# A fused attention and two-layer MoE kernel: the first MoE's first product by seven block products instead of eight, with the second product two pairs behind

## The reference

```python
def sm_attn(qq, kk, vv):
    s = scale * np.matmul(qq, kk.transpose(0, 1, 3, 2))
    s = s - np.max(s, axis=-1, keepdims=True)
    a = np.exp(s)
    a = a / (np.sum(a, axis=-1, keepdims=True) + 1e-09)
    return np.matmul(a, vv)
p_packed = sm_attn(p, k, v)               # batch 8, heads 8, 32 packed queries, keys 576, head_dim 64
x = sm_attn(q, p_packed, p_packed)        # then laid out as 4608 tokens x 512

h = x @ w_in                              # first MoE: 512 -> 2048
x1 = (h - np.tanh(h)) @ w_out             # 2048 -> 512
h = x1 @ w_in2                            # second MoE
r = np.maximum(h, 0.0)
y = (s * (r * r) + b) @ w_out2
```

## Time and profile before

| | us |
|---|---|
| median of 3 runs (lowest to highest) | 1444.14 (1443.78 to 1445.14) |
| the profiled execution's own time | 1444.17 |
| its span, first to last instruction | 1442.3 |
| PE, DVE, ACT busy in the span | 1431.0, 826.2, 548.2 |

### The profile page before, as it was taken

How to read it: one execution, slowest core, us unless ns; L and a number is a source line. 1 busy time by engine, 2 the same in 40 slices (tenths; PEclk the granted TensorE clock), 3 DMA queues, 4 the chain that set the end, 5 groups by cost and what they waited for, 6 DMA issues and landing times.

```text
span 1442.3 us, 22038 instructions
## 1 busy us (share of the span) xinstructions
PE 1431.0 (99%) x8584; PEld 1189.7 (82%) x8584; DVE 826.2 (57%) x1442; ACT 548.2 (38%) x996; POOL 78.0 (5%) x71
## 2 busy tenths in 40 slices
PE   8999999999999999999999999999999999999998
PEld 6788887878788888888898888888888888888887
DVE  7565555555555555764667455844557455754553
ACT  3444343443443343443344223722235223632243
POOL 2242010100101000000000000000000000000000
PEclk9999999999999999999999999999999999999999
DMA  9898777687877754668697644865466644756145
GB/s 347 283 309 298 237 239 267 226 289 234 276 251 255 241 179 148 225 231 286 232 360 271 240 166 180 280 227 220 180 235 234 254 170 174 279 214 245 59 131 190
DMA packets 128807, 337.51 MB, mean 234 GB/s; under 512 B 22976, under 2 KB 46656, under 8 KB 124096
## 3 DMA queue, kind: packets, MB, share of 16 engines
q1 hardware_dynamic: 128560, 336.04, 66.5%
q10 hardware_dynamic: 144, 0.07, 0.0%
HBM read 282.07 MB, written 54.00 MB: 233 GB/s over the span
## 4 chain that ended last, share of the span: by engine, by line
PE 97%; DMA 1%; DVE 1%; SPq 0%; ACT 0%; issue 0%; DVEq 0%; ACTq 0%
PE banks L304 31%; PE banks L305 31%; PE banks L306 30%; PE banks L675 2%; DMA qT<-q_T 1%; PE banks L617 1%; PE banks L639 1%; PE banks L694 1%; PE banks L625 0%; SPq L362 0%; ACT g_high L933 0%; DVE g L1308 0%; DVE w_in_first L1249 0%; PE banks L603 0%; PE banks L648 0%
## 5 line engine op out<-in xcount | busy, mean ns | idle before, releaser
L304 PE MATMUL banks<-g_high,w_out_ring 128*128 128x512 f32 x1152 | 456.8, 397 | 0.4 <-DVE g_low L1232 0.4
L305 PE MATMUL banks<-g_low,w_out_ring 128*128 128x512 f32 x1152 | 449.3, 390 | 0.0
L306 PE MATMUL banks<-g_high,w_out_ring 128*128 128x512 f32 x1152 | 448.7, 390 | 0.0
L304 PEld LDWEIGHTS banks<-g_high,w_out_ring 128*128 128x128 f32 x1152 | 216.3, 188 | 73.1 <-issue 15.8
L306 PEld LDWEIGHTS banks<-g_high,w_out_ring 128*128 128x128 f32 x1152 | 216.4, 188 | 46.1
L305 PEld LDWEIGHTS banks<-g_low,w_out_ring 128*128 128x128 f32 x1152 | 216.5, 188 | 40.1
L1308 DVE TENSOR_TENSOR g<-banks,tanh 128x288 f32<-128x288 f32 x256 | 115.9, 453 | 232.2 <-ACT tanh L973 231.9
L1033 ACT ACTIVATE g<-g,small 128x512 f32<-128x512 f32 x144 | 117.4, 815 | 295.0 <-DVE g L1398 294.3
L973 ACT ACTIVATE tanh<-banks 128x288 f32<-128x288 f32 x256 | 105.4, 412 | 281.2 <-PE banks L306 279.1
L304 PE MATMUL banks<-x_operands_wide,w_in_first 128*128 128x512 f32 x448 | 174.3, 389 | 0.0
L305 PE MATMUL banks<-x_operands_wide,w_in_first 128*128 128x512 f32 x448 | 174.3, 389 | 0.0
(11 more groups left out here) (146 smaller groups left out, 1458.2 us busy)
## 6 DMA issues: line engine op xcount, KB each, us to landing
w_out_ring<-w_out_parts_scratch SPq DMA_DIRECT2D x272, 512.0 KB, 4.1
w_in_first<-w_in_operands_scratch SPq DMA_DIRECT2D x28, 1792.0 KB, 7.3
w_in_ring<-w_in SPq DMA_DIRECT2D x30, 1024.0 KB, 6.4
kT<-k_T SPq DMA_DIRECT2D x16, 576.0 KB, 7.0
qT<-q_T SPq DMA_DIRECT2D x16, 576.0 KB, 5.9
x1T_scratch<-out_store SPq DMA_DIRECT2D x9, 1024.0 KB, 7.5
v_rows<-v_rows SPq DMA_DIRECT2D x8, 1024.0 KB, 6.5
w_out_parts_scratch<-w_out_ring SPq DMA_DIRECT2D x16, 512.0 KB, 4.7
```

Source lines behind the costliest of these rows:

```text
L304: nc.tensor.matmul(out, high, rhigh, start=first, stop=False)
L305: nc.tensor.matmul(out, high, rlow, start=False, stop=False)
L306: return nc.tensor.matmul(out, low, rhigh, start=False, stop=last)
```

## The change

The loop over steps becomes a loop over 64 pairs of feature chunks (8 in a batch; p is the pair, q its place in the batch). The first four pairs are done as before, with 16 steps called `plain`. In each of the other 60 the 2x2 blocks (two inner blocks, two chunks by two inner blocks, two token halves) go by seven products instead of eight, 21 matmuls of 288 columns instead of 24. Of these:

- the operands are seven blocks each, made by DVE: for M in `m_round` and `m_sums` (in two pairs `m_round` once and `m_sums` twice), for the softmax weights in `at_mix` and `at_lows` (once in a batch);
- the products are summed partly in PSUM: ACT copies the first product from bank 4 to bank 6 (`move_p1`), a product is added on top, ACT copies that to bank 7 (`move_u2`), and the next are added on both. The product in bank 5 is copied to SBUF (`copy_p5`) and DVE adds it in (`add_pair`);
- the second product runs two pairs behind, `second_d` giving its four output blocks one at a time between the seven products; g is kept in a ring of four pairs, and every pair's leftover tokens are stored on their own;
- banks 4 to 7 are all taken by the pair, so the side work (`side`, `side_late`) borrows banks 4 and 5 between the last product of one pair and the first of the next, and `side_free` makes PE wait until they are read.

```diff
+LAG = 2
+            def side_late(p):
+                b, q = divmod(p, PF)
+                if q == 1 and b + 1 < B:
+                    pe.wait_ge(turn2_done, 2 * b + 2)
+                    if b + 2 < B:
+                        pe.wait_ge(s1_out, s1_copied(b + 2) + 2)
+                    scores2(2 * b + 3)
...
+                if q == 7 and b + 2 < B:
+                    if b + 3 < B:
+                        pe.wait_ge(s1_out, s1_copied(b + 3) + 1)
+                    packed_t(2 * b + 4)
+                    packed_t(2 * b + 5)
+            def pair(p):
...
+                side_free(p - 1, C11)
+                prod(C11, 0, 0, True, True).then_inc(p1_done, 1)
+                second_d(a, 0)
+                pe.wait_ge(p1_moved, k + 1)
+                pe.wait_ge(mb_ready, 4 * n + 3 + p % 2)
+                prod(U2B, 4, 5, False, True).then_inc(u2_done, 1)
+                prod(C11, 1, 1, False, True).then_inc(c11_done, 1)
+                second_d(a, 1)
+                pe.wait_ge(u2_moved, k + 1)
+                wait(pe, p5_copied, k)
+                side_free(p - 1, P5)
+                prod(P5, 3, 4, True, True).then_inc(p5_done, 1)
+                prod(U3B, 5, 6, False, True).then_inc(p7_done, 1)
+                prod(U2B, 6, 3, False, True).then_inc(p3_done, 1)
+                second_d(a, 2)
+                second_d(a, 3)
+                pe.wait_ge(add_done, 2 * k + 1)
+                prod(U3B, 2, 2, False, True).then_inc(p4_done, 1)
+                side(p)
+                second_d(a + 1, 0)
+                second_d(a + 1, 1)
+                second_d(a + 1, 2)
+                side_late(p)
+                second_d(a + 1, 3)
...
+            def move_p1(p):
...
+                nc.scalar.copy(banks[:, U2B, 0:U1], banks[:, C11, 0:U1]).then_inc(p1_moved, 1)
...
+                move_p1(p)
+                high_g1(2 * (p - 1))
+                move_u2(p)
+                tanh_pair(p, 0)
+                high_g1(2 * (p - 1) + 1)
+                copy_p5(p)
+                if q % 2 == 1 and (p - 1) // 2 + 1 < ROUNDS and p > PLAIN:
+                    m_sums((p - 1) // 2 + 1, 0)
+                    m_sums((p - 1) // 2 + 1, 1)
+                if b + 1 < B and q == 3:
+                    exp2(nxt)
+                for i in range(1, 4):
+                    tanh_pair(p, i)
...
+                low_g1(2 * (p - 1))
+                minus_pair(p, 0)
+                low_g1(2 * (p - 1) + 1)
...
+                if 1 <= b < B - 1 and q == 2:
+                    max2_(nxt)
+                    sub2(nxt)
+                if 1 <= b < B - 2 and q == 4:
+                    max1(nxt + 2)
+                    max1(nxt + 3)
+                add_pair(p)
+                for i in range(1, 4):
+                    minus_pair(p, i)
```

1027 lines of the change are left out of this document (607 added, 420 removed).

## The result

The changed kernel takes 1528.78 us (median of 4, 1523.22 to 1532.7) against 1444.57 (1443.78 to 1445.14) for the kernel before in the same comparison: ratio 1.058, 95% interval 1.0544 to 1.0617. It is 84 us slower, where 32 were forecast. The profiled execution has a span of 1529.7 us.

The account below looks back on a forecast made before the run. PE's work, busy 1431.0 of 1442.3 us, was taken to bound the kernel. 1442.3 - 23.9 removed + 53 of waits + 3 at the start = 1474.4 of span, 1476 with the 1.9 around it; range 1452 to 1490.

Parts of the forecast that it names:

- The matmuls removed: On PE, 60 pairs lose three matmuls of 288 columns, 0.1325 us each: 23.9 us saved, 3.2 in a batch.
- DVE's work: Per batch, DVE gets 21 us more than 43.5, about 65 where PE needs 76.8; fits on average.
- Rival 3: Bank copy or PSUM traffic is dear: `move_p1` at 0.6 us bites in 60 pairs, 18 more, 1494; chance 0.06.
- Places A to C: Three spots in a batch where PE waits behind softmax work; with 0.3 at q = 6, 7.6 us a full batch.
- B: Pair q = 7, batches 0 to 4: PE waits 2.1 us before the packed rows' transposes, 0.15 more behind them.
- place A: Pairs q = 3 and 4, batches 1 to 5: softmax work on DVE delays the addition; PE waits 2.7 us.
- Rival 4: The clock falls in pauses, each under 3 us; a batch at 1.2 GHz would add some 77; chance 0.02.
- The ninth block: End of the first MoE's second product: no wait of its own; second product and transfers costed at nothing.
- The start: Before pair 4, M's low parts share VectorE with the softmax: 3 us more waiting, between 0 and 8.
- The pairs: Waits in the 60 changed pairs: 8.9 us in batch 0, 7.6 each in batches 1 to 4; 53 in all.
- Range: Whole kernel: 1452 to 1490 us, reaching over most of rival 2 and some way towards rival 3.
- Rival 2: Half the waits: ACT and DVE overlap more, or a place is misplaced; 27 to 38 us, 1447 to 1461; chance 0.15.

Follow-up runs that it names:

- adds_first: Changed kernel with softmax maxima and subtraction on VectorE put behind the additions and subtractions in pairs 2 and 4 of each full batch; 1508.88 us, ratio 1.0448.
- norms_first: Changed kernel with `norm1` ahead of `m_sums` in pair 7 and `at_lows` moved to the end of pair 6 on VectorE; 1508.46 us, ratio 1.0444.
- hold_sooner: Changed kernel plus useless TensorE products inside the pauses of pairs 4 and 7, the latter ahead of the scores copy wait; 1519.88 us, ratio 1.0519.
- all_orders: Changed kernel with `adds_first`, `norms_first`, earlier left-column loads, later x-operand work in the ninth block, and `turn2` ahead of `m_sums` in pair 1; 1480.54 us.
- best: `all_orders` plus a GpSimd wait before the fifth w_out split, earlier low parts of the start's last weight pair, and useless products in batch 0's pauses; 1477.16 us.
- after_again: The changed kernel itself measured once more, nothing edited; 1526.57 us, ratio 1.0569 against the kernel before.
- left_only: Changed kernel with only the loads of g's left columns issued two second products earlier; 1524.37 us, ratio 1.0565.

## Why the prediction was wrong

The direction and the mechanism were right, the size was not: 1528.8 is outside 1452 to 1490. Step by step, on the span (1529.7 against the forecast's 1474.4, 55 too few):

- *The matmuls removed, 3 x 0.1325 in a pair.* Right in its kind, 0.34 instead of 0.40. The last pairs of the last batch wait for nothing. In the kernel before, TensorE, the same matmul four steps (one pair of chunks) apart; in the changed kernel, the bank copy of two pairs in turn:

```profile
623.34 0.29 PE L304 MATMUL banks<-probs2T_parts,m_parts 128*128 128x288 f32 x1
...
631.99 0.29 PE L304 MATMUL banks<-probs2T_parts,m_parts 128*128 128x288 f32 x1
```

```profile
700.66 0.38 ACT L1099 COPY banks<-banks 128x288 f32<-128x288 f32 x1 [2.72 <-PE banks L844]
...
708.97 0.38 ACT L1099 COPY banks<-banks 128x288 f32<-128x288 f32 x1 [1.05 <-PE banks L844]
```

  8.65 against 8.31, and 8.25 was walked. Over 60 pairs that is 20, not 24.
- *DVE's work.* Right in sum: 293.8 us of busy time from 140 to 540, or 65 in a batch of 88.6, as forecast. The bank copies take 0.388 and 0.383 and the copy of product 5 to SBUF 0.402 (0.40 was taken), the additions 0.449 and 0.446. Rival 3 falls with them. The Trainium skill's rule on ScalarE's destinations (ScalarE: Activation LUTs, what happens step by step) has the sign right, by 0.014 to 0.019 us. What was mis-sized is `low_g1` in pair 4, 0.71 in the prediction and up to 1.42 beside GpSimd, which has no term in it.
- *Places A to C, 7.6 a batch.* Right in place, order and nearly in size: 85.4 us a batch with the clock held, against 84, and `adds_first` and `norms_first` shorten A and take B away by moving the instructions that were named. In place A TensorE went on at 8.7 us into the pair (265.69 less 257.03) where 7.8 were walked: the two `low_g1` and the subtraction between them took 2.6 us (260.85 to 263.50) instead of 1.6.
- *Rival 4, the clock, 0.02.* This step failed first. It was said that the granted clock keeps its level through the start's waits for loads, and so through pauses under 3 us. But in the kernel of the earlier trace rows the longest pause of TensorE is 1.05 us, at the very start, so it says nothing on pauses of 1.6 to 2.5. The shape was wrong too: I priced a batch at 1.2 GHz, 77 us, where the falls last some 3.4 us, longer in places, and cost 1.2 to 1.8 each. `hold_sooner` measures 3.2 in a batch, and 6.7 to 8.9 us in all for batches 1 to 4; batch 0, the start and the ninth block have their own, and are not separated here.
- *The ninth block, at nothing.* This step failed most. "The transfers (same bytes; the ring's loads stay four chunks ahead)" is true of w_out, but the change replaced `load_left` into a full G by `load_left` into two slots and left `mix_x` in VectorE's queue close behind the last pair, where it waited 11 us for its transfers. 15.5 us: 70.5 against the 55.0 that `all_orders` needs.
- *The start, 3 us, 0 to 8.* Too little. What the forecast of the second MoE's start (730.2) and the measured 784.3 leave, after 15.5 in the ninth block and 28.0 in the pairs (my walk has 615 us from pair 4's first to pair 63's last matmul, and 643.0 were measured), is 10.6 more. The 615 is worked out from the prediction's terms and stands nowhere in it; how the loss divides between the start and the pairs rests on it. In rows there are 5.1 us of waits for `m_operands` L1352, where before they were 0.6, and 3.8 us of slowed `at_lows` and `m_sums`; how these and the low clock between 30 and 38 us divide the 10.6 stays open.
- *The pairs, 28 us more than walked.* 8 of them in the four pairs of batch 0, which took 56.4 instead of 48.1, about 16 in batches 1 to 4 (88.6 for 84.4 each), of which the held clock gives back 3.2 each and GpSimd in pair 4 has most of the rest. The 8 of batch 0 are not explained by a run: `best`, with holds there and the clock at 0.95 from 60 to 100 us and 1.00 from 100 to 140, gained 1.4 us over `all_orders` in all the pairs, so most of it isn't the clock. GpSimd, which is at work for 28 of the 80 us from 60 to 140, is a candidate that no run tests: the three `at_lows` of pair 7 take 4.29 us beside it, against 2.39 in a steady batch.
- *Range.* I let it end at 1490 because the waits were counted row by row; the terms that failed most, the clock, the start and the ninth block, were ones that I hadn't counted row by row. "At nothing" was given to stages in which the change had moved transfers and queue places. Rival 2's bounds don't fit together either: 27 us of waits without the start's 3 give 1447, and 38 with them 1461.

## What to carry over

A table of averages that says an engine has room (here 65 of 77 us) says nothing on the next instruction in its queue: walk each place where a short result is wanted soon behind long work that nobody waits for, and put the wanted one first. Where a change first makes TensorE pause, price the clock as well, from a profile in which it pauses, and from more than one execution, since the same pauses bring it down in one and not in the next. Don't add up what two mended pauses gave one by one. Look at GpSimd too where a chain on VectorE is walked: an engine that TensorE never waits for can still lengthen the instruction that it does wait for. Give "at nothing" only to a stage whose queues you have read as closely as the loop's; the last block, where rings drain and the next stage's loads begin, is one of the places where a wait at the head of a queue is longest.

## What the runs showed of the hardware

- The granted clock can be at its lower level, 1.2 GHz, for some 3.4 us behind a pause of 1.6 to 2.5 us, and the same pause of 1.58 us brings it down in some batches and executions of one kernel and not in others: in pair 7 of batches 1 to 4, four times of four in the changed kernel's profile, two of four in `after_again`, none of four in `left_only`.
- A batch of the same code takes 85.1 to 85.6 us with the clock at 1.00, 86.8 to 87.7 at 0.98 and 88.5 to 89.1 at 0.96.
- Matmuls without use keep it up: from 140 to 540 us it is 1.00 in every stretch of `hold_sooner`, and the result is 6.7 to 8.9 us faster.
- VectorE and GpSimd slow each other where both work from SBUF to SBUF: 512 columns took 1.60 us on VectorE instead of 0.64 apart, and GpSimd's 1.04 us became 1.60 to 1.85. In pair 4 of batches 1 to 4 `low_g1` takes up to 1.42 us so, against 0.65 to 0.68 in batch 5.
- A ScalarE copy of 288 columns from one PSUM bank to another takes 0.383 to 0.388 us, to SBUF 0.402.
